# Windowed attention woven into the first MLP, one beat of it for each weight chunk, with the odd weight chunks fetched again for each tile

## What is computed

```python
scores = scale * np.matmul(q, k.transpose(0, 1, 3, 2))
mask = (rel >= 0) & (rel < window)                      # window = 128
scores = np.where(mask, scores + bias[None], -1000000000.0)
attn = np.exp(scores - np.max(scores, axis=-1, keepdims=True))
attn = attn / (np.sum(attn, axis=-1, keepdims=True) + 1e-09)
x = np.matmul(attn, v)                                  # (B, H, S, D) -> (2304, 512)
h = x @ w_in                                            # 512 -> 2048
x = (s * np.maximum(h, 0.0) ** 2 + b) @ w_out           # 2048 -> 512
logits = x @ w_gate
noisy_logits = logits + np.log1p(np.exp(x @ w_noise)) * noise
top2 = np.argpartition(-noisy_logits, 2, axis=1)[:, :2]
...
    h = np.maximum(x[mask] @ w1[e], 0.0)                # expert e: 512 -> 1024 -> 512
    out[mask] += top2_w[mask, k, None] * (h @ w2[e])
```

## Time and profile before

| | us |
|---|---|
| median of 3 runs (1247.77 to 1251.87) | 1250.87 |
| span of the profiled execution | 1249.5 |
| PE busy in it | 1122.7 (90%) |
| attention, 0 to 252 us | 252 |
| first MLP, 252 to 688 us | 436 |
| last routing and table, 688 to 720 us | 32 |
| experts, 720 us to the end | 529.5 |

### The profile page before, as it was taken

How to read it: one execution, slowest core, us unless ns; L and a number is a source line. 1 busy time by engine, 2 the same in 40 slices (tenths; PEclk the granted TensorE clock), 3 DMA queues, 4 the chain that set the end, 5 groups by cost and what they waited for, 6 DMA issues and landing times.

```text
span 1249.5 us, 21689 instructions
## 1 busy us (share of the span) xinstructions
PE 1122.7 (90%) x6799; PEld 987.4 (79%) x6800; DVE 692.3 (55%) x1999; ACT 412.4 (33%) x949; POOL 301.6 (24%) x210
## 2 busy tenths in 40 slices
PE   3776666789999999999999299999999999999996
PEld 3555455579989888898888189999999999999995
DVE  7999999952334344433435564546364545446332
ACT  3655555522223232323322141423141413223121
POOL 4455555430001010010273111211121211211111
PEclk8888887789999999999999699999999999999998
DMA  9455555588002010020132151426152433525222
GB/s 226 132 148 148 147 154 158 160 256 326 26 1 77 0 51 25 0 76 0 51 100 85 68 163 57 136 86 201 45 191 75 152 105 112 175 72 164 78 80 87
DMA packets 80900, 137.27 MB, mean 110 GB/s; under 512 B 11372, under 2 KB 24876, under 8 KB 80864
## 3 DMA queue, kind: packets, MB, share of 16 engines
q1 hardware_dynamic: 68640, 111.36, 29.6%
q0 software_dynamic: 9920, 20.78, 4.8%
q10 hardware_dynamic: 2304, 4.72, 1.1%
HBM read 97.15 MB, written 51.49 MB: 119 GB/s over the span
## 4 chain that ended last, share of the span: by engine, by line
PE 76%; DVE 1%; DMA 1%; POOL 0%; issue 0%; ACT 0%; POOLq 0%; DVEq 0%
PE bank L1142 24%; PE bank L1143 24%; PE bank L1144 24%; PE bank L1229 2%; PE bank L1170 1%; PE bank L1163 1%; DVE x_lo L846 1%; POOL rows_scratch L698 0%; DMA x_raw<-rows_scratch 0%; DMA rows_scratch<-x,slot 0%; POOLq L611 0%; PE bank L1178 0%; DVE x L970 0%; ACT L761 0%; DVEq L611 0%
## 5 line engine op out<-in xcount | busy, mean ns | idle before, releaser
L1142 PE MATMUL bank<-x_hi,w_hi 128*128 128x256 f32 (+1 forms) x896 | 274.1, 306 | 7.3 <-DVE x_lo L846 5.8
L1144 PE MATMUL bank<-x_hi,w_lo 128*128 128x256 f32 (+1 forms) x896 | 272.3, 304 | 0.0
L1143 PE MATMUL bank<-x_lo,w_hi 128*128 128x256 f32 (+1 forms) x896 | 272.1, 304 | 0.0
L1143 PE MATMUL bank<-w_lo,g_hi 128*128 128x512 f32 x526 | 207.5, 395 | 0.0
L1142 PE MATMUL bank<-w_hi,g_hi 128*128 128x512 f32 x526 | 207.5, 394 | 0.0
L1144 PE MATMUL bank<-w_hi,g_lo 128*128 128x512 f32 x526 | 206.4, 392 | 0.0
L853 DVE SCALAR_TENSOR_TENSOR squared<-relu,sb_scale 128x384 f32<-128x384 f32 x96 | 63.1, 657 | 235.7 <-ACT relu L747 234.8
L1142 PEld LDWEIGHTS bank<-x_hi,w_hi 128*128 128x128 f32 x896 | 172.1, 192 | 16.9 <-issue 5.9
L815 ACT ACTIVATE g_hi<-bank 128x256 fp32r<-128x256 f32 x176 | 67.7, 385 | 347.7 <-PE bank L1144 329.2
L1143 PEld LDWEIGHTS bank<-x_lo,w_hi 128*128 128x128 f32 x896 | 172.3, 192 | 6.1
L1100 DVE SCALAR_TENSOR_TENSOR g_lo<-bank,g_hi 128x256 fp32r<-128x256 f32 x176 | 74.5, 424 | 183.2 <-ACT g_hi L815 183.2
(11 more groups left out here) (160 smaller groups left out, 1886.9 us busy)
## 6 DMA issues: line engine op xcount, KB each, us to landing
y_scratch<-x SPq DMA_DIRECT2D x41, 512.0 KB, 6.4
stage<-in_w_first SPq DMA_DIRECT2D x80, 256.0 KB, 3.2
stage<-in_w_second SPq DMA_DIRECT2D x80, 256.0 KB, 4.1
x_raw<-rows_scratch SPq DMA_DIRECT2D x23, 516.0 KB
k_raw<-in_kT SPq DMA_DIRECT2D x36, 288.0 KB, 5.3
q_raw<-in_qT SPq DMA_DIRECT2D x36, 288.0 KB, 5.9
xT_scratch<-xo ACTq DMA_DIRECT2D x16, 288.0 KB, 5.2
x_raw<-xT_scratch SPq DMA_DIRECT2D x24, 192.0 KB, 3.3
```

The lines of the kernel that those rows point to most:

```text
L1142: pe.matmul(psum, lh, rh, start=(first and n == 0), stop=False)
L1143: pe.matmul(psum, lh, rl, start=False, stop=False)
L1144: done = pe.matmul(psum, ll, rh, start=False, stop=(last and n == len(pairs) - 1))
```

## The change

Attention works on 18 blocks of 128 tokens of the joined sequences (`NB`), 4 pairs of heads each, so 72 units (called *beats*). A block that crosses from one sequence to the next gets a `seam` product that masks the other sequence. A beat `i` holds on PE the scores of unit `i` and the transposes of unit `i - 2`; on DVE `add_bias(i)`, `normalise(i - 1)` and the low halves of the queries and keys of the next block's unit (`rest_of_qk`); on ACT `exps(i)`, `copy_t(i - 2)` and the high halves of that unit (`split`). In every fourth beat PE weighs the values of a whole block (`weigh_values`), ACT writes the block's `x_hi` and DVE its `x_lo`, straight from PSUM, without a trip to DRAM.

The first 15 beats (`LEAD`) run alone. The rest are put into the slots of the MLP, one beat into each of slots 0, 1, 2, 4, 5, 6, 8, 9, 10, 12, 13 and 14 of tiles 0 to 4 (`beat_at`).

SBUF no longer holds all 16 chunks. Eight even ones stay in `w_hi`, `w_lo`; the odd ones go through two places, `w_now`, and are loaded and halved again for each tile. `round_at` says in which slot: in tile 0 chunk `c + 2` in slot `c`; in later tiles chunk 3 in slot 1, chunks 5, 7, ..., 15 in slots 4, 6, ..., 14, chunk 1 of the next tile in slot 16. In the last tile the first expert's eight chunks are put in too, in slots 3, 5, ..., 17. The halving is ACT's copy (`round_weights`) and DVE's difference (`rest_of_weights`), both at the end of the slot on their engines; POOL halves nothing any more. The zeroing of `rows_scratch` and `y_scratch` is spread over slots 2 to 11 of tile 0. The ACT table is loaded once, and `x2T` is copied by ACT instead of DVE. The experts' stage is unchanged but for names.

```diff
-        w_hi = sb("w_hi", [P, C1 - LATE, CW], F32R)
-        w_lo = sb("w_lo", [P, C1 - LATE, CW], F32R)
-        stage = sb("stage", [P, STAGES, CW], F32)
+        w_hi = sb("w_hi", [P, C2, CW], F32R)
+        w_lo = sb("w_lo", [P, C2, CW], F32R)
...
+def beat_at(t, c):
+
+    if t == T1 - 1 or c >= C1 or c % 4 == 3:
+        return None
+    return LEAD + 12 * t + 3 * (c // 4) + c % 4
...
+def round_at(t, c):
...
+    if t == 0 and c < C1 - 2:
+        p = c + 2
+        return p, p, p, (p - 4 if p % 2 and p >= 4 else None)
+    last = t == T1 - 1
+    if c == C1 and not last:
+        return C1 + t * (C1 // 2), 1, 1, t * C1 + 13
+    if t == 0:
+        return None
+    first = C1 + (t - 1) * (C1 // 2)
+    p = 3 if c == 1 else c + 1 if c % 2 == 0 and 4 <= c <= 14 else None
+    if p is not None:
+        return first + (p - 1) // 2 + ((p - 3) // 2 if last else 0), p, p, t * C1 + p - 4
+    if last and (c % 2 and 3 <= c):
+        e = min((c - 3) // 2, C2 - 1)
+        return (first + 2 + 2 * e if e < C2 - 1 else SROUNDS - 1), C1 + e, C1 + e, t * C1 + 2 * e
+    return None
...
+def round_of(t, p):
+
+    if t == 0 or p % 2 == 0:
+        return p
+    return C1 + (t - 1) * (C1 // 2) + (p - 1) // 2 + ((p - 3) // 2 if t == T1 - 1 and p >= 3 else 0)
...
+        def ring_a(half, p):
+
+            if p >= C1:
+                return (w_hi, w_lo)[half][:, p - C1, :]
+            return w_now[half][:, p // 2 % 2, :] if p % 2 else (w_hi, w_lo)[half][:, p // 2, :]
...
+        def load_round(sp, r):
+
+            if r >= EARLY:
+                sp.wait_ge(w_ready, r - EARLY + 1)
+            load_weights(sp, chunk_of(r), r % EARLY)
...
+                for t in range(T1):
+                    for c in range(C1 + LAG):
+                        if beat_at(t, c) is not None:
+                            beat(beat_at(t, c))
+                        if round_at(t, c) is not None and round_at(t, c)[0] + EARLY < SROUNDS:
+                            load_round(sp, round_at(t, c)[0] + EARLY)
...
+                def split(n, hp):
...
+                    act.wait_ge(raw_in[hp], (n + 1) * 32)
+                    if n >= 1:
+                        act.wait_ge(s_ready, 4 * (n - 1) + hp + 1)
+                    act.activation(qk_hi[:, i, hp], qk_raw[:, hp], ACT.Copy).then_inc(qk_hi_done, 1)
...
+                def exps(i):
+                    keys, hp = keys_of(i // HP)[0], i % HP
+                    act.wait_ge(biased, i + 1)
...
+                def x_of_block(n):
+                    t, j = n // BLK1, n % BLK1
+                    act.wait_ge(pv_done, n + 1)
...
+                    act.activation(x_hi[t % 2][:, :, j * P:(j + 1) * P],
+                                   o_bank[:].rearrange("p (h q) -> p h q", h=HP), ACT.Copy).then_inc(xh_ready, 1)
...
+                def beat(i):
+                    if i < UNITS:
+                        exps(i)
+                    if i >= WEIGH and (i - WEIGH) % HP == 0:
+                        x_of_block((i - WEIGH) // HP)
+                    if 0 <= i - TURN < UNITS:
+                        copy_t(i - TURN)
+                    if i // HP + 1 < NB:
+                        split(i // HP + 1, i % HP)
+
+                def round_weights(r, p, use):
+                    act.wait_ge(stage_full[r % EARLY], (r // EARLY + 1) * 32)
+                    if use is not None:
+                        act.wait_ge(chunk_used, use + 1)
+                    act.activation(ring_a(0, p), stage(r % EARLY), ACT.Copy).then_inc(w_hi_done, 1)
...
-                def mlp_tile(t, routed):
-                    for c in range(C1 + 1):
+                act.preload_act_table_set("natural_log_exp_and_others")
+                for hp in range(HP):
+                    split(0, hp)
...
+                for t in range(T1):
+                    for c in range(C1 + LAG):
+                        if t >= 1 and c == 0:
+                            copy_out(t - 1)
                         if c < C1:
                             relus(t, c)
-                        if c >= 1:
+                        if 1 <= c <= C1:
                             round_g(t, c - 1)
-                        if routed is not None and c == 8:
-                            softplus(routed)
-                        if routed is not None and c == 10:
-                            second_weight(routed)
-
...
+                        if t >= 1 and 1 <= c <= BLK1:
+                            copy_x2T(t - 1, c - 1, o_bank)
+                        if beat_at(t, c) is not None:
+                            beat(beat_at(t, c))
+                        if round_at(t, c) is not None:
+                            r, _, p, use = round_at(t, c)
+                            round_weights(r, p, use)
...
+                def after_scores(i):
+                    if 0 <= i - 1 < UNITS:
+                        normalise(i - 1)
+                    if i // HP + 1 < NB:
+                        rest_of_qk(i // HP + 1, i % HP)
+                    if i >= WEIGH and (i - WEIGH) % HP == 0:
+                        rest_of_x((i - WEIGH) // HP)
+
+                def rest_of_weights(r, p):
+                    dve.wait_ge(w_hi_done, r + 1)
+                    dve.tensor_tensor(ring_a(1, p), stage(r % EARLY), ring_a(0, p).bitcast(F32), ALU.subtract
+                                      ).then_inc(w_ready, 1)
...
-                def mlp_tile(t, routed):
-                    for c in range(C1 + 1):
-                        if c < C1:
-                            square(t, c)
-                        if c >= 1:
-                            rest_of_g(t, c - 1)
-                        if routed is not None:
-                            if c == 4:
...
+                for t in range(T1):
+                    for c in range(C1 + LAG):
+                        if t >= 1 and c == 0:
+                            copy_out(t - 1)
+                        i = beat_at(t, c)
+                        if i is not None and i < UNITS:
+                            add_bias(i)
+                        if t >= 1 and c == 4:
+                            copy_logits(t - 1, t_bank)
+                        if c < C1:
+                            square(t, c)
+                        if 1 <= c <= C1:
+                            rest_of_g(t, c - 1)
+                        if i is not None:
+                            after_scores(i)
+                        if round_at(t, c) is not None:
+                            rest_of_weights(round_at(t, c)[0], round_at(t, c)[2])
+                        if t >= 1 and c == 7:
+                            choose(t - 1, o_bank)
+                        if t >= 1 and c == 11:
+                            assign(t - 1)
...
+                def weigh_values(n):
+                    blocks = keys_of(n)[2]
+                    pe.wait_ge(v_in[n % VS], (n // VS + 1) * 16)
+                    pe.wait_ge(t_copied, HP * n + HP)
+                    if n >= 1:
+                        pe.wait_ge(xl_ready, n)
...
-                def mlp_tile(t, routed):
+                def mlp_slot(t, c, i):
...
+                        before_mlp(i)
+                    if c < C1:
+                        if c == 0:
...
+                        if t * C1 + c >= 2:
+                            pe.wait_ge(relu_ready, t * C1 + c - 1)
+                        pe.wait_ge(w_ready, round_of(t, c) + 1)
+                        first_product((ring_a(0, c), ring_a(1, c)), (x_hi[t % 2], x_lo[t % 2]), TOK1,
+                                      h_bank[c % 2]).then_inc(h_ready, 1)
+                    if i is not None:
...
+                        after_mlp(i)
+                    if c >= LAG:
+                        g = c - LAG
...
+                        pe.wait_ge(g_ready, t * C1 + g + 1)
+                        second_product((ring_a(0, g), ring_a(1, g)), (t * C1 + g) % GR, BLK1, g == 0, g == C1 - 1
+                                       ).then_inc(chunk_used, 1)
...
+                pe.wait_ge(ident_in, 16)
+                for i in range(LEAD):
+                    before_mlp(i)
+                    after_mlp(i)
+                for t in range(T1):
...
-                        if c < C1:
-                            if c >= 2:
-                                pe.wait_ge(relu_ready, t * C1 + c - 1)
-                            pe.wait_ge(w_ready, c + 1)
...
-                mlp_tile(0, None)
-                pe.wait_ge(const_done, 2)
-                with pe.Fori(1, T1) as t:
-                    mlp_tile(t, t - 1)
```

More of the change, by code:

```diff
@@ L1136, in _, with scores @@
             def _(pe):
-                def three(psum, pairs, first, last, before=None):
+                def scores(i):
+                    n, hp = i // HP, i % HP
+                    keys, own = keys_of(n)[0], n % SEQ % 2
+                    held = slice(0, keys // P)
+                    pe.wait_ge(qk_ready, i + 1)
+                    if i > FREE:
+                        pe.wait_ge(biased, i)
+                    elif i == FREE:
```

(36 more changed lines are left out.)

920 lines of the change are left out of this document (399 added, 521 removed).

## The result

The changed kernel takes **1273.65 us** in the median of 4 runs (1271.30 to 1276.68), the kernel before 1249.98 in the same comparison: a ratio of 1.0197, 95% interval 1.0173 to 1.022. It is slower by 24 us; the prediction was 1277 (1225 to 1300).

What follows compares the result with a forecast made beforehand. DVE bounds attention, PE the MLP and experts. Lead 79.3, tile 0 96, tiles 1 to 4 441.6, clock 16, last tile 81.8, routing 31.2, experts 529.5: span 1275.4, plus 1.4, gives 1277 us; range 1225 to 1300.

Steps and rivals of the forecast that it cites:

- 15 beats in front: Attention beats before the MLP: 3.8 us for an ordinary beat, 79 us in all, bounds 70 and 88.
- tile 0: First MLP tile: no chunk waited for, 87 us, plus slow first slots 4, weighing 2, zeroing writes 3; 96.
- tiles 1 to 4, waits for the chunk: PE waits before slots 5, 7, 9, 11, 13 and 15 for the odd chunk's halving: 16.0 us a tile, 64 total.
- tiles 1 to 4, low clock: Some waits leave PE at 1.2 GHz, each costing 1.7 us: 3.9 us a tile, 16 in four.
- tiles 1 to 4, all else: PE's work, 92.0 us a tile if nothing waits, plus 2.4 of other waits; 377.6 in four tiles.
- last tile: MLP tile without beats: 71.7 us, six waits of 1.46 for chunks (8.8) and 1.3; 81.8.
- The chain of 5.5 us: From the slot's first product's end through ACT's queue and DVE's difference to PE: 5.5 us against 2.6 of PE work.
- Rival 3: The odd chunk's halving is hidden behind PE's queued work, so its waits and clock loss vanish: 1188 us; chance 0.17.
- The wait before slot 9: PE's wait for the odd chunk there in tiles 1 to 4, mostly covered by weighing: 0.8 us.
- rival 1: All five waits above 2 us in a tile drop the clock: 34 us instead of 16, 1295; chance 0.13.
- eight "fast restarts": Attention in the kernel before: eight of seventeen waits read as restarting at full clock, three after more than 3.2 us.
- The routing's two DVE chains: Routing work on DVE in slots without beats: costed at nothing; if not covered, up to 1 us each.

Runs made afterwards that it cites:

- the first experiment: Against the changed kernel, the halving in tiles 1 to 5 stands at the front of the slot on ACT and DVE; 1181.37 us, ratio to before 0.9456.
- the kernels with the shorter lead: Changed kernel with halving at slot front and ACT's split ahead of the exponentials in the lead, 1169.52 us; then also the y_scratch zeroing moved into the lead, 1162.42 us.
- two other kernels: Changed kernel with only ACT's copy of the odd chunk moved to the slot's front, 1261.77 us; changed kernel with last-tile routing one slot later, 1269.73 us.

## Why the prediction was right, step by step

| stage | forecast us | measured us |
|---|---|---|
| 15 beats in front | 79.3 | 77.04 |
| tile 0 | 96 | 98.9 |
| tiles 1 to 4, waits for the chunk | 64 | 52.5 |
| tiles 1 to 4, low clock (measured: all extra busy time) | 16 | 27.9 |
| tiles 1 to 4, all else | 377.6 | 366.2 |
| last tile | 81.8 | 86.9 |
| last routing | 31.2 | 30.8 |
| experts | 529.5 | 529.2 |
| span | 1275.4 | 1269.4 |

(The three rows of tiles 1 to 4 are measured as differences to the first experiment: idle time, busy time, and what is left there.)

**The cause** stands as forecast. Moving the halving within its slot, and nothing else, removes 92 us; two half-way positions give the waits that the same sum of rows gives, 60 and 24 us forecast, 60.5 and 25.0 measured. The chain of 5.5 us was read right to 0.02 us in the slot shown above. Rival 3, the hidden halving, is what the first experiment makes true, and would have been the right forecast for a kernel with that order.

**The waits** were 56.4 us in the trace instead of 64, and 52.5 net of the small waits of the first experiment (10.4 us there, 6.5 beside these). The unit that splits is four ahead, so the last splits are in the fifth beat of tile 4, and from there on the chain lacks 0.5 us of ACT and 0.85 of DVE: tile 4 has 11.4 us of these waits where tile 1 has 14.8. I had given every tile the same 16.0. The wait before slot 9, forecast at 0.8, was 0.26 in tile 1.

**The clock** is the step that failed in size. "Of the ten waits of 3.2 to 3.9 us there, seven end at the lower level; of seven between 2 and 3 us, two" judged each wait by the matmul right behind it, while the drop comes up to 1.4 us later. Read by a stretch of windows, 15 of the 18 waits over 2 us here cost the clock, and the 16 should have been about 25 (15 times the prediction's own 1.7): half way to rival 1, whose 34 had all twenty waits. The other 3.4 of the 27.9 are restarts at the full clock, which the forecast did not have. The Trainium skill, TensorE: Matmul & The Clock Gate, section "HAM oscillation — how this bites in real kernels", tells of a kernel whose waits of some 3 to 5 us leave the next burst slow, every time. I held the eight "fast restarts" against it; six of them were misreadings, three of these behind waits over 3.2 us. With 15 drops in 18 the trace is near to the page, though not at every time; and nine of the 15 follow waits of 2.3 to 2.9 us, shorter than those it tells of.

**All else in a tile**: a tile without these waits takes 91.5 us, forecast 92.0 and 2.4 of other waits. Too much by 2.9 a tile; four tiles give the 11.4. Together with the waits this is what hid the error in the clock: -11.4, -11.5 and +11.9. The total was right to 6 us of span, partly by luck.

**The last tile** was forecast with six equal waits of 1.46 us. Four measured 1.3; those before slots 9 and 13 measured 2.25 and 2.76. "The routing's two DVE chains" stand in the way in this tile. I had costed them at nothing and named up to 1 us each; they cost 0.9 and 1.4, and the first one 1.7 of clock as well. Put a slot later, they give back 4 of the 5 us by which the tile was longer than forecast.

**Tile 0** lost 6.7 us to the zeroing of `y_scratch` (in the kernels with the shorter lead, where this was measured), forecast 3 within 0 to 10. **The lead** came out 2.3 us shorter.

**DVE with little of POOL beside it**: as forecast, `total_eps` stays near 160 ns; its longest instruction is 360 ns where the earlier trace rows shows 2544.

```profile
L699 DVE TENSOR_SCALAR total_eps<-total x72: 155/161/360, 16.0 to 598.4; 128x2 f32<-128x2 f32 x72
```

In the kernel before, 24 of the 80 take 0.9 to 2.5 us, and each of these starts while a tensor instruction of POOL runs. The longest, and POOL beside it:

```profile
27.84 2.54 DVE L365 TENSOR_SCALAR total_eps<-total 128x2 f32<-128x2 f32 x1
27.71 2.64 POOL L138 TENSOR_TENSOR k_lo<-k_raw,k_hi 128x1152 fp32r<-128x1152 f32 x1 [4.87 <-DVE k_hi L347]
```

No run takes only POOL's work away, so this stays what two traces show beside each other.

## What to carry to other kernels

Weaving one stage into another frees no time while a load that the next slot needs is prepared at the *end* of a queue that serves both. Sum that queue from the event that starts it and compare it with the work that the waiting engine has in stock; then look whether the step can stand ahead of that event, since an engine that idles there takes it for nothing. When you price a wait of PE, look at the granted clock over the five us behind it, not at the first matmul; and compare busy time only between kernels with as many restarts.

## What the runs showed of the hardware

- In tiles 1 to 4 of the changed kernel TensorE's clock fell at 15 of 18 waits of 2.3 to 3.8 us, nine times only 0.15 to 1.4 us after work had begun again, otherwise at the restart or up to 0.9 us before it; it stayed low for 3.4 us, once for 6.8. In two other kernels it was 11 of 16 and 14 of 18.
- Waits for the chunk of 0.2 to 1.6 us left the clock at 1.00 in all four tiles of two kernels (halving in the middle; wait filled).
- Of 80 small DVE instructions of 0.16 us those 24 that took 0.9 to 2.5 us all began during a tensor instruction of POOL.
- Useless matmuls in a wait can pay: 20 fills of 2.1 us made the changed kernel 24.6 us faster.
- Where PE waits often, its busy time isn't constant. The same matmuls of tiles 1 to 4 were busy 383.7 us in the changed kernel, 359.2 with short waits at the full clock and 355.8 with hardly any, and a sum that takes only idle time for loss leaves out a third of it here (27.9 of 80.4).
